# Splitting q and k after the transpose instead of before it, and storing the last output tiles one by one

## The chip, the core and the metric

The kernel runs on one core of one Trainium2 chip. The metric is the device time of one execution in microseconds (us). A core has five engines that run their own instruction streams and meet on semaphores: TensorE (PE, matrix products and transposes), VectorE (DVE), ScalarE (ACT), GpSimd (POOL) and SyncE (SP, which here only issues transfers). SBUF is the on-chip memory with 128 partitions, PSUM the eight banks into which PE writes.

## What is computed

A block-causal attention, then a mixture of eight experts with a skip test, then a two-layer MLP, all in float32:

```python
def _attn_ref(q, k, v):            # 4 batches, 8 heads, 576 tokens, 64 dims a head
    scores = scale * np.matmul(q, k.transpose(0, 1, 3, 2))
    scores = np.where(block_i >= block_j, scores, -1000000000.0)   # blocks of 64
    scores = scores - np.max(scores, axis=-1, keepdims=True)
    attn = np.exp(scores)
    attn = attn / (np.sum(attn, axis=-1, keepdims=True) + 1e-09)
    return np.matmul(attn, v)
...
# x = attention output, 2304 tokens x 512
# experts: out = x, or x + gate * relu(x @ w1[e]) @ w2[e] where x @ w_skip > 0
# MLP: g = max(h, 0) + alpha * min(h, 0), h = x @ w_in (512 x 2048);  out = g @ w_out
```

## The kernel before, in words

The 32 heads are taken as 16 pairs of heads. A pair has nine units (`UNITS`): four query tiles of 128 tokens of each of the two heads (`FULL`), and a joint unit (`JOINT`) for the last 64 queries of both heads (`TAIL`). A unit is scores on PE (L739 and the mask at L741, or L733 for the joint one), a maximum on DVE (L1117), an exponential on ACT (L976), transposes of the probabilities on PE (L751) and a copy of them on DVE (L1131, L1128). Once a pair, PE multiplies with v (L762, L768) for the pair before and turns the output back to rows (L786); DVE sums up (L1137 to L1142) and scales.

Scores need near-float32 precision from a PE format that rounds (`F32R`). So q and k are split into a rounded part (high) and the rest (low), and each score is two products of depth 128: high and low parts of one head are stacked on the two halves of the partitions, keys as (high, low), queries once as (high, low) and once swapped as (low, high).

Before the change, GpSimd splits q and k **as loaded**, tokens on partitions (`split_pair`: additions of zero at L579 give the high part, subtractions at L583 the low part), into `parts`, where each tile of each head is 64 columns high and 64 columns low. PE transposes these 128x128 tiles (`qk_chunk`, L715 for full tiles, L711 for the tails), 18 in a pair: 4 of q and 4 of k for each head, and 2 tails. They come in the five chunks of `CHUNKS`, at units 2, 3, 3, 5 and 6 of the pair ahead of the one that uses them (`QK_AT`), into a ring of three PSUM banks (`RING`, in the order of `ORDER`) shared with the transposed probabilities. ACT copies them out (`qk_out`, L962 to L967) into `q_t` and `k_t`. The swapped queries are made by SP with transfers from SBUF to SBUF (`swap`, L417), four in a pair of 160 KB each.

The order on every engine is written out by hand: `pair(n, par)` on PE, ACT and DVE. SP's queue has in each step (`load_step(n)`) the loads of q and k for pair n+2 (six transfers), the swaps of head 0 of pair n+1, the three loads of v, the swaps of head 1, and behind them one transfer each that zeroes, saves finished rows (in the later steps) and loads expert weights (in the first eight steps). SP waits in that order, so what stands behind a waiting transfer waits too.

The MLP goes in six chunks of three tiles. At its end, `project` signals `g_used` after the last nine products (L931), ACT copies three tiles (`out_rows`, L1095) and SP stores them (L536, L540).

## Time and profile before

| what | us |
|---|---|
| median of 3 runs (lowest, highest) | 872.41 (871.15, 872.70) |
| the profiled execution | 871.87 |
| its span, first to last instruction | 870.0 |
| attention stage (scores of all 16 pairs), about | 0 to 234 |
| routing, about | 234 to 255 |
| experts, about | 255 to 430 |
| MLP, about | 430 to 870 |
| PE busy in the span | 817.1 |
| DVE, ACT, POOL busy | 446.4, 274.5, 190.4 |

The busy times of the engines overlap. A pair of the attention stage takes 13.7 us, so the stage is sixteen nearly equal periods with a start and an end.

### The profile page before, as it was taken

How to read it: one execution, taken by the hardware profiler on the slowest of the kernel's cores; microseconds unless marked ns; L12 is line 12 of the kernel's file. 1: busy time of each engine (PE TensorE's matmuls, PEld its weight loads, DVE VectorE, ACT ScalarE, POOL GpSimd, SP SyncE). 2: the span in 40 equal slices, each digit the busy share in tenths (PEclk: the TensorE clock that was granted, in tenths of full speed). 3: DMA queues.
4: the chain of work that ended last, by engine and by line, in shares of the span. 5: the costliest groups of instructions: out<-in, count | busy, mean ns of one | idle time of the engine just before them, and what ended most of it. 6: DMA issues, size and time to landing. Idle time of an engine off the chain costs nothing.

```text
span 870.0 us, 15697 instructions
## 1 busy us (share of the span) xinstructions
PE 817.1 (94%) x5281; PEld 721.9 (83%) x5282; DVE 446.4 (51%) x916; ACT 274.5 (32%) x650; POOL 190.4 (22%) x191
## 2 busy tenths in 40 slices
PE   5999999999749999999769999999999999999997
PEld 4788888888549989989659889989998998998996
DVE  3777777777874444226544734543544434444432
ACT  5666665666333333133311121111112112112111
POOL 6242424422011143014178810000001001000000
PEclk9999999999959999999969999999999999999999
DMA  6678888675417766149433110002002002000001
GB/s 140 160 188 222 215 229 234 164 208 166 141 39 242 273 234 227 50 169 323 148 108 99 60 44 29 0 2 70 0 0 72 0 0 72 0 0 36 1 1 37
DMA packets 94599, 95.76 MB, mean 110 GB/s; under 512 B 64112, under 2 KB 65264, under 8 KB 94064
## 3 DMA queue, kind: packets, MB, share of 16 engines
q1 hardware_dynamic: 86000, 67.65, 27.4%
q0 software_dynamic: 4208, 14.95, 5.8%
q10 hardware_dynamic: 4368, 12.88, 4.0%
q8 instruction: 12, 0.20, 0.1%
q14 instruction: 11, 0.09, 0.0%
HBM read 64.78 MB, written 20.19 MB: 98 GB/s over the span
## 4 chain that ended last, share of the span: by engine, by line
PE 86%; DVE 4%; DMA 3%; ACT 3%; issue 2%; POOL 0%; SPq 0%; ACTq 0%; DVEq 0%; POOLq 0%
PE bank L920 23%; PE bank L931 22%; PE bank L870 9%; PE bank L884 8%; PE bank L751 6%; PE bank L762 4%; PE bank L739 3%; PE bank L715 2%; PE bank L733 2%; PE bank L786 2%; DMA w_sb<-in_moe_w_dram 1%; ACT p_sb L976 1%; PE bank L768 1%; PE bank L908 1%; PE bank L857 1%
## 5 line engine op out<-in xcount | busy, mean ns | idle before, releaser
L1412 DVE TENSOR_SCALAR g_sb<-bank,alpha_sb 128x384 f32<-128x384 f32 x96 | 59.3, 618 | 218.7 <-PE bank L920 218.6
L1088 ACT CAST g_hi<-g_sb 128x384 fp32r<-128x384 f32 x96 | 49.5, 515 | 321.8 <-DVE g_sb L1414 321.8
L920 PE MATMUL bank<-u_hi,wi_hi 128*128 128x384 f32 x384 | 130.5, 340 | 1.4 <-DVE u_lo L1385 1.4
L920 PE MATMUL bank<-u_hi,wi_lo 128*128 128x384 f32 x384 | 130.4, 340 | 0.0
L920 PE MATMUL bank<-u_lo,wi_hi 128*128 128x384 f32 x384 | 130.0, 339 | 0.0
L931 PE MATMUL bank<-wo_lo,g_hi 128*128 128x512 f32 x288 | 113.7, 395 | 0.0
L931 PE MATMUL bank<-wo_hi,g_lo 128*128 128x512 f32 x288 | 113.5, 394 | 0.0
L931 PE MATMUL bank<-wo_hi,g_hi 128*128 128x512 f32 x288 | 112.7, 391 | 0.8 <-DVE g_lo L1418 0.8
L870 PEld LDWEIGHTS bank<-rows_t,w_sb 128*128 128x128 f32 x832 | 97.6, 197 | 2.6 <-DVE rows_t L1329 1.5
L870 PE MATMUL bank<-rows_t,w_sb 128*128 128x128 f32 x832 | 97.9, 280 | 1.1 <-DVE rows_t L1329 1.1
L976 ACT ACTIVATE p_sb<-bank,neg_max 128x128 f32<-128x128 f32 (+2 forms) x144 | 79.1, 551 | 48.6 <-DVE neg_max L1117 46.1
L1117 DVE TENSOR_REDUCE neg_max<-bank 128x1 f32<-128x128 f32 (+2 forms) x144 | 72.5, 511 | 33.4 <-PE bank L733 19.3
L920 PEld LDWEIGHTS bank<-u_hi,wi_hi 128*128 128x128 f32 x384 | 73.0, 190 | 5.4 <-DVE u_lo L1385 1.8
L920 PEld LDWEIGHTS bank<-u_lo,wi_hi 128*128 128x128 f32 x384 | 72.9, 190 | 3.6
L920 PEld LDWEIGHTS bank<-u_hi,wi_lo 128*128 128x128 f32 x384 | 72.9, 190 | 0.0
L751 PE MATMUL bank<-ident,p_sb 128*128 128x128 f32 x400 | 69.3, 285 | 1.8 <-DVE p_t L1131 0.3
L739 PE MATMUL bank<-k_t,q_t 128*128 128x128 f32 (+3 forms) x256 | 68.0, 358 | 2.2 <-DMA q_t<-q_t 1.4
L1131 DVE COPY p_t<-bank 128x128 f32<-128x128 f32 (+3 forms) x128 | 60.6, 484 | 14.6 <-PE bank L751 12.9
L660 POOL DMA_INDIRECT u_sb<-y_slots,from_i x18 | 18.2, 1010 | 227.8 <-PE bank L908 214.4
L931 PEld LDWEIGHTS bank<-wo_lo,g_hi 128*128 128x128 f32 x288 | 54.0, 188 | 11.6
L931 PEld LDWEIGHTS bank<-wo_hi,g_hi 128*128 128x128 f32 x288 | 54.1, 188 | 10.4 <-issue 1.3
L931 PEld LDWEIGHTS bank<-wo_hi,g_lo 128*128 128x128 f32 x288 | 54.0, 188 | 9.1
(171 smaller groups left out, 1230.2 us busy)
## 6 DMA issues: line engine op xcount, KB each, us to landing
w_sb<-in_moe_w_dram ACTq DMA_DIRECT2D x6, 2048.0 KB, 8.0
w_sb<-in_moe_w_dram SPq DMA_DIRECT2D x6, 2048.0 KB, 10.8
q_t<-q_t SPq DMA_DIRECT2D x64, 160.0 KB, 2.5
w_sb<-in_moe_w_dram SPq DMA_DIRECT2D x16, 512.0 KB, 4.8
v_nat<-in_v_dram SPq DMA_DIRECT2D x32, 128.0 KB, 2.4
y_out<-in_moe_w_out_dram POOLq DMA_DIRECT2D x16, 256.0 KB, 3.0
out_dram<-y_out SPq DMA_DIRECT2D x16, 256.0 KB, 2.8
qk_nat<-in_q_dram SPq DMA_DIRECT2D x30, 128.0 KB, 4.0
```

The lines of the kernel that those rows point to most:

```text
L739: pe.matmul(a[:, 0:keys], q_t[:, par, z, h, P * (i + 1):P * (i + 2)], k_t[:, par, h, 0:keys], start=z == 0, stop=False)
L751: last = pe.transpose(t[:, P * j:P * j + P], p_sb[:, c % PB, P * j:P * j + P], ident[:])
L762: last = pe.matmul(O_MAIN[HALF * h:HALF * h + HALF, P * unit:MAIN], v_nat[:, unit, h, :], p_t[:, h, unit, P * unit:MAIN], start=unit == 0, ...
L870: last = pe.matmul(HIDDEN[c][:, P * z:P * z + P], w1_sb[:, par, j, P * f:P * f + P], rows_t[:, j, :], start=j == 0, stop=j == KD - 1)
L884: last = pe.matmul(RESULT, h[:, f, :], w, start=f == 0 and z == 0, stop=f == KF - 1 and z == 2)
L920: last = pe.matmul(dst, w[:, j, P * f:P * f + P], u[:, j, :], start=z == 0, stop=z == len(terms) - 1)
L931: last = pe.matmul(YBANK[i][:, :], g[:, f % GB, P * i:P * i + P], w[:, f, :], start=f == 0 and z == 0, stop=f == FI - 1 and z == 2)
L976: act.activation(p_sb[:, c % PB, 0:keys], scores_ap(c), ACT.Exp, bias=neg_max[:, c:c + 1], accum_out=row_sum[:, par, i, h:h + 1]).then_inc ...
L1088: act.copy(g_hi[:, f % GB, :], g_sb[:, f % 2, :]).then_inc(g_hi_done, 1)
L1117: dve.reduce_max(neg_max[:, c:c + 1], scores_ap(c), AX.X, negate=True).then_inc(max_done, 1)
L1131: dve.tensor_copy(p_t[:, h, 0:i + 1, P * i:P * i + P], t[:, 0:P * (i + 1)].rearrange("p (j c) -> p j c", c=P)).then_inc(pt_evac, 1)
L1412: dve.tensor_scalar(g, a, 0.0, alpha_sb[:, f:f + 1], ALU.min, ALU.mult).then_inc(neg_done, 1)
```

## The change

q and k are transposed as they are loaded: a 128x128 tile holds both heads, 64 columns each, so a pair has 9 transposes (4 of q, 4 of k, 1 for the tails), in three chunks at units 2, 3 and 5. They are made two pairs ahead. ACT copies them as plain float32 into `raw_t`; GpSimd then splits them there, a pair ahead, one head at a time on the 64 partitions of that head (four instructions of 64x1152), into `qk_t`. SP brings the missing halves over: for each head first the high part of q (64x576), then the low parts of q and k (64x1152). Pair 0 is split by ACT and DVE directly from PSUM. `qk_nat` gets two buffers, `parts` goes. In the last MLP chunk PE signals after each tile's three products, ACT copies each tile when it is ready, and ACT itself issues the last half tile's store.

```diff
-        CHUNKS = [(0, 0), "tails", (0, 1), (1, 0), (1, 1)]
+        CHUNKS = ["q", "k", "tails"]
...
-        QK_AT = [2, 3, 3, 5, 6]
+        QK_AT = [2, 3, 5]
+        GAP_AT = [3, 6]
...
+            def swap(n, par, h):
+
+                sp.wait_ge(hi_done, 2 * n - 1 + h)
+                sp.dma_start(columns(other(h), n, LOW_AT[h], S).bitcast(F32), high(n, h)[:, 0:S].bitcast(F32)
+                             ).then_inc(swapped[par][h], 16)
+                sp.wait_ge(lo_done, 2 * n - 1 + h)
+                sp.dma_start(columns(other(h), n, HIGH_AT[h], 2 * S).bitcast(F32), low(n, h).bitcast(F32)
+                             ).then_inc(swapped[par][h], 16)
+
+            def load_step(n, par, more=True):
+
+
+                if more:
+                    sp.wait_ge(qk_tr, QC * n + QC)
+                    load_qk(n + 3, 1 - par)
+                swap(n + 1, 1 - par, 0)
                 sp.wait_ge(pv_done, 2 * n)
                 load_v(n)
-                swap(n + 1, (1,))
+                swap(n + 1, 1 - par, 1)
...
             first_load(sp, 0, q_h)
-            load_qk(1, first_nat, second_loaded)
+            load_qk(1, 1)
+            swap_first(0)
+            load_half(2, 0, 0)
+            swap_first(1)
+            load_half(2, 1, 0)
             sp.wait_ge(v_zero, 1)
             load_v(0)
-            swap(0)
-            sp.wait_ge(first_split, 2)
-            load_qk(2, qk_nat, qk_loaded)
-            swap(1)
+            sp.wait_ge(qk_tr, QC)
+            load_qk(3, 1)
+            swap(1, 1, 0)
+            swap(1, 1, 1)
...
+            def split_pair(n, par, second=False):
+
+                pool.wait_ge(qk_evac, QC * n)
+                if not second:
+                    pool.wait_ge(s_done, UNITS * (n - 1))
+                for h in range(2):
+                    src = raw_t[own(h), par]
+                    pool.tensor_tensor(high(par, h), src, zero_c[own(h), :].to_broadcast([HALF, 2 * S]), ALU.add).then_inc(hi_done, 1)
+                    pool.wait_ge(hi_done, 2 * n - 1 + h)
+                    pool.tensor_tensor(low(par, h), src, high(par, h).bitcast(F32), ALU.subtract).then_inc(lo_done, 1)
...
+            def turn(src, c, t):
+
+                tiles = {"q": range(FULL), "k": range(FULL, 2 * FULL), "tails": [2 * FULL]}[CHUNKS[c]]
+                for i, z in enumerate(tiles):
+                    last = pe.transpose(t[:, P * i:P * i + P], src[:, z].rearrange("p h d -> p (h d)"), ident[:])
+                return last
...
+            def project_end(c):
+
+                f = FI - 1
+                pe.wait_ge(g_lo_done, FI * c + FI)
+                for i in range(CH):
+                    for z, (g, w) in enumerate(((g_hi, wo_hi), (g_lo, wo_hi), (g_hi, wo_lo))):
+                        last = pe.matmul(YBANK[i][:, :], g[:, f % GB, P * i:P * i + P], w[:, f, :], start=False, stop=z == 2)
+                    last.then_inc(last_done, 1)
```

**PE in the middle of a pair (units 2 and 3).** In the rows, bank and bank_4 are banks of the ring, `parts` is what GpSimd split, `p_sb` the probabilities, `k_t,q_t` the operands of the scores. Before:

```order
L715 MATMUL bank<-ident,parts 128x128 x4
L739 MATMUL bank_2<-k_t,q_t 128x256 x2
L741 MATMUL bank_2<-mask_r,mask_l 128x64
L749 REGISTER_ALU
L751 MATMUL bank_4<-ident,p_sb 128x128 x4
L711 MATMUL bank_4<-ident,parts 128x128 x2
L702 ISA
L715 MATMUL bank<-ident,parts 128x128 x4
```

The same place in the changed kernel, where L759 is the transpose of the loaded q and k and L793, L795, L805 are the former L739, L741, L751:

```order
L759 MATMUL bank<-ident,qk_nat 128x128 x4
L793 MATMUL bank_2<-qk_t 128x256 x2
L795 MATMUL bank_2<-mask_r,mask_l 128x64
L803 REGISTER_ALU
L805 MATMUL bank_4<-ident,p_sb 128x128 x4
L759 MATMUL bank_4<-ident,qk_nat 128x128 x4
```

The two tail transposes have left this place, one has gone to unit 5, and the chunks of four at units 5 and 6 are gone.

**GpSimd, one pair.** Before:

```order
L579 TENSOR_TENSOR parts<-qk_nat,zero_c 128x8x64
L579 TENSOR_TENSOR parts<-qk_nat,zero_c 128x10x64
L581 REGISTER_ALU
L583 TENSOR_TENSOR parts<-qk_nat,parts 128x8x64
L583 TENSOR_TENSOR parts<-qk_nat,parts 128x10x64
```

In the changed kernel the four instructions of a pair have 1152 columns each on 64 partitions:

```order
L628 TENSOR_TENSOR qk_t<-raw_t,zero_c 64x1152
L629 ISA
L630 TENSOR_TENSOR qk_t<-raw_t,qk_t 64x1152
L628 TENSOR_TENSOR qk_t<-raw_t,zero_c 64x1152
L630 TENSOR_TENSOR qk_t<-raw_t,qk_t 64x1152
```

The columns that go through the engine rise from 2304 to 4608 a pair.

**SP at the start of the program**, from the load of v for pair 0 to the swaps of pair 1. Before (the first L417 row is pair 0's four swaps, the second pair 1's):

```order
L401 DMA v_nat<-in_v_dram 128x4x64 x2
L404 DMA v_nat<-in_v_dram 64x2x64
L417 DMA q_t<-q_t 64x640 x4
L393 DMA qk_nat<-in_q_dram 128x4x64 x2
L396 DMA qk_nat<-in_q_dram 64x2x64
L393 DMA qk_nat<-in_k_dram 128x4x64 x2
L396 DMA qk_nat<-in_k_dram 64x2x64
L417 DMA q_t<-q_t 64x640 x4
```

In the changed kernel, from pair 0's swaps of head 1 (L445, L448) to pair 1's of head 0 (L454, L457); ahead of it stand the swaps of head 0 and pair 2's load of q:

```order
L445 DMA qk_t<-qk_t 64x576
L448 DMA qk_t<-qk_t 64x576
L424 DMA qk_nat<-in_k_dram 128x4x64 x2
L427 DMA qk_nat<-in_k_dram 64x2x64
L436 DMA v_nat<-in_v_dram 128x4x64 x2
L439 DMA v_nat<-in_v_dram 64x2x64
L424 DMA qk_nat<-in_q_dram 128x4x64 x2
L427 DMA qk_nat<-in_q_dram 64x2x64
L424 DMA qk_nat<-in_k_dram 128x4x64 x2
L427 DMA qk_nat<-in_k_dram 64x2x64
L454 DMA qk_t<-qk_t 64x576
L457 DMA qk_t<-qk_t 64x1152
```

Pair 1's swaps now stand behind the loads of two more pairs and of v.

## Rows read from the trace of the kernel before

**Rows 1.** Busy time by stretch: start:end, length, busy us of each engine (instructions), clock, DMA share, GB/s.

```profile
94.80:108.50 13.70, 13.61 (x124) 11.35 (x122) 9.96 (x28) 8.76 (x27) 5.05 (x4) 1.00 0.88 227
```

**Rows 2.** The chain that ended last, one pair: start us, us, what.

```profile
121.74 2.35 PE bank L762 x16
...
125.73 0.44 PE bank L715 x4
...
126.92 0.23 PE bank L711 x2
...
129.16 0.44 PE bank L715 x4
129.59 1.29 PE bank L733 x8
...
131.24 0.44 PE bank L715 x4
...
135.46 2.35 PE bank L762 x16
```

**Rows 3.** GpSimd by form, 45 to 205 us: count, busy us, mean ns, idle before.

```profile
L583 POOL TENSOR_TENSOR parts<-qk_nat,parts 128x640 fp32r<-128x640 f32 x12 | 18.6, 1549 | 0.0
...
L579 POOL TENSOR_TENSOR parts<-qk_nat,zero_c 128x640 fp32r<-128x640 f32 x12 | 15.0, 1253 | 0.0
```

**Rows 4.** Timeline of GpSimd at the start: start us, us, engine, line, operation.

```profile
1.74 0.14 POOL L554 MEMSET mask_l<- 1x64 bf16 x1
...
1.82 0.14 POOL L555 MEMSET mask_r<- 128x64 bf16 x1
```

**Rows 5.** The chain that ended last, at the start of the program.

```profile
5.59 0.86 DVE parts L1209
...
7.31 1.10 PE bank L715 x4
...
10.07 2.59 DMA q_t<-q_t
...
12.80 0.41 PE bank L739 x2
```

**Rows 6.** Timeline of SP and PE at the start (SPq is SP's queue issuing transfers).

```profile
12.38 1.19 SPq L393 DMA_DIRECT2D qk_nat<-in_q_dram  x2
...
15.11 0.42 PE L739 MATMUL bank<-k_t,q_t 128*128 128x128 f32 x2
...
22.02 0.42 PE L739 MATMUL bank<-k_t,q_t 128*128 128x128 f32 x2
```

**Rows 7.** Timeline of SP over one period.

```profile
100.46 1.28 SPq L417 DMA_DIRECT2D q_t<-q_t  x2
...
111.70 1.36 SPq L396 DMA_DIRECT2D qk_nat<-in_k_dram  x1
```

**Rows 8.** Busy time of one microsecond in which swaps of rows 7 run.

```profile
102.00:103.00 1.00, 1.00 (x9) 0.88 (x7) 0.28 (x1) 0.79 (x2) 0.71 (x1) 1.00 0.95 220
```

**Rows 9.** Timeline of the end.

```profile
864.35 1.56 ACT L1095 COPY y_out<-bank 128x512 f32<-128x512 f32 x3 [4.41 <-PE bank L931]
864.96 0.33 SPq L536 DMA_DIRECT2D out_dram<-y_out  x1
865.45 2.40 SPq L540 DMA_DIRECT2D out_dram<-y_out  x4
```

**Rows 10.** Single DVE lines: count, duration ns min/median/max, first and last start us.

```profile
L1398 DVE SCALAR_TENSOR_TENSOR u_sb<-u_sb,gate,x_tok x15: 740/747/2017, 482.6 to 762.3; 128x512 f32<-128x512 f32 x15
```

**Rows 11.** Timeline of GpSimd and DVE in one pair.

```profile
131.95 2.77 POOL L583 TENSOR_TENSOR parts<-qk_nat,parts 128x512 fp32r<-128x512 f32 x2
...
137.33 0.15 DVE L1137 TENSOR_SCALAR sum_eps<-row_sum 128x8 f32<-128x8 f32 x1
...
138.77 0.62 DVE L1131 COPY p_t<-bank 128x128 f32<-128x128 f32 x2 [0.81 <-PE bank L751]
```

**Rows 12.** Busy time in one microsecond of routing.

```profile
237.00:238.00 1.00, 0.00 (x0) 0.00 (x0) 0.90 (x4) 0.00 (x0) 0.00 (x0) 0.65 0.00 0
```

**Rows 13.** The chain that ended last, two experts' first layers.

```profile
255.22 10.24 PE bank L870 x64
...
271.50 7.14 PE bank L870 x64
```

More of the change, by code:

```diff
@@ L43, in program @@
     NAT = 2 * FULL + 1
-    QW = P + MAIN
     UNITS = 2 * FULL + 1
@@ L375, in program, with turns, own, other @@
         SAVED = 16 * ((B - 1) * FULL + B - 1 + 4)
+        FIRST_BANKS = [bank[7], bank[3], bank[2]]
+        SECOND_BANKS = [bank[5], bank[6], bank[4]]
+        def turns(n):
+            return not isinstance(n, int) or n + 2 < PAIRS
+        def own(h):
+            return slice(HALF * h, HALF * h + HALF)
+        def other(h):
+            return slice(HALF - HALF * h, P - HALF * h)
+        def columns(rows, n, at, count):
+            if isinstance(n, int):
+                return qk_t[rows, n % 2, at:at + count]
+            return qk_t[rows, bass.ds(n % 2, 1), at:at + count].rearrange("p a s -> p (a s)")
+        def high(n, h):
+            return columns(own(h), n, HIGH_AT[h], 2 * S)
+        def low(n, h):
+            return columns(own(h), n, LOW_AT[h], 2 * S)
         def first_load(queue, z, src):
             for h in range(2):
-                queue.dma_start(qk_nat[:, FULL * z:FULL * z + FULL, h, :],
+                queue.dma_start(first_nat[:, FULL * z:FULL * z + FULL, h, :],
                                 src[h:h + 1, 0:MAIN, :].rearrange("a (t p) d -> p (a t) d", p=P)
                                 ).then_inc(first_loaded[z], 16)
-            queue.dma_start(qk_nat[TAIL * z:TAIL * z + TAIL, 2 * FULL, :, :],
+            queue.dma_start(first_nat[TAIL * z:TAIL * z + TAIL, 2 * FULL, :, :],
                             src[0:2, MAIN:S, :].rearrange("h p d -> p h d")).then_inc(first_loaded[z], 16)
@@ L537, in _ @@
                     else:
-                        for z in range(2):
+                        for z in range(1 if t == T_TILES - 1 else 2):
                             b = 2 * (t - B * FULL) + z
@@ L558, in _ @@
             pool.memset(o_t[:, S:], 0.0).then_inc(ident_0, 1)
-            for h in range(2):
-                pool.memset(q_t[:, :, 0, h, HALF - HALF * h:P - HALF * h].bitcast(F32), 0.0).then_inc(ident_0, 1)
+            for at in (HIGH_AT[1], LOW_AT[1]):
+                pool.memset(qk_t[:, :, at - HALF:at].bitcast(F32), 0.0).then_inc(ident_0, 1)
             pool.memset(w_route[:], 0.0).then_inc(route_zero, 1)
@@ L815, in _ @@
             pair(0, 0, first=True)
-            with pe.Fori(1, PAIRS - 1, 2) as n:
+            with pe.Fori(1, PAIRS - 3, 2) as n:
                 pair(n, 1)
                 pair(n + 1, 0)
+            pair(PAIRS - 3, 1)
+            pair(PAIRS - 2, 0)
             pair(PAIRS - 1, 1, last=True)
@@ L994, in pair @@
                     for j, at in enumerate(QK_AT):
-                        if at == c - 1 and not last:
+                        if at == c - 1 and turns(n):
                             qk_next(j, n, par)
@@ L1000, in _ @@
             act.activation(warm[:], zero_c[:], ACT.Exp)
-            act.wait_ge(first_loaded[0], 48)
-            act.wait_ge(first_loaded[1], 48)
-            act.copy(parts[:, 0, FULL:, :, 0:DH], qk_nat[:, FULL:]).then_inc(first_hi, 1)
+            first_high()
+            for c in range(QC):
+                qk_out(c, 1, 1, SECOND_BANKS[c])
             act.wait_ge(const_ready, 1)
-            for c in range(QC):
-                qk_out(c, 0, 0, RING[(c - QC) % 3])
             pair(0, 0, first=True)
-            with act.Fori(1, PAIRS - 1, 2) as n:
+            with act.Fori(1, PAIRS - 3, 2) as n:
                 pair(n, 1)
                 pair(n + 1, 0)
+            pair(PAIRS - 3, 1)
+            pair(PAIRS - 2, 0)
             pair(PAIRS - 1, 1, last=True)
@@ L1095, in out_rows, with last_rows @@
                     act.copy(y_out[:, i, :], YBANK[i][:, :]).then_inc(out_evac, 1)
+            def last_rows(c):
+                act.wait_ge(wo_split, FI)
+                act.wait_ge(out_stored, 16 * CH * c + 16)
+                for i in range(CH):
+                    act.wait_ge(last_done, i + 1)
+                    act.copy(y_out[:, i, :], YBANK[i][:, :]).then_inc(out_evac, 1)
+                act.wait_ge(out_evac, CH * c + 2 * CH)
+                act.dma_start(out[B * S - TAIL:B * S, :], y_out[P - TAIL:P, CH - 1, :]).then_inc(last_stored, 16)
             def mlp_step(c, last):
@@ L1206, in _ @@
             dve.sem_inc(head_part_done, 1)
[L1208 to L1215 removed]
+            for h in range(2):
+                dve.wait_ge(first_hi, 2 * h + 1)
+                for lo, hi, src in ((TAIL, S, FIRST_BANKS[0][:, 0:MAIN]), (0, TAIL, FIRST_BANKS[2][:, 0:TAIL])):
+                    last = dve.scalar_tensor_tensor(low(0, h)[:, lo:hi], src[own(h)], SCALE, high(0, h)[:, lo:hi].bitcast(F32),
+                                                    ALU.mult, ALU.subtract)
+                last.then_inc(first_lo, 1)
+                dve.wait_ge(first_hi, 2 * h + 2)
+                k_low = columns(other(h), 0, HIGH_AT[h] + S, S)
+                for lo, hi, src in ((TAIL, S, FIRST_BANKS[1][:, 0:MAIN]), (0, TAIL, FIRST_BANKS[2][:, TAIL:2 * TAIL])):
+                    last = dve.tensor_tensor(k_low[:, lo:hi], src[own(h)], high(0, h)[:, S + lo:S + hi].bitcast(F32), ALU.subtract)
+                last.then_inc(first_lo, 1)
             dve.wait_ge(ones_ready, 1)
```

266 lines of the change are left out of this document (130 added, 136 removed).

## The prediction

> **What bounds the kernel now.** I read the busy time by stretch first. In a period of the attention stage PE is busy for 13.61 of 13.70 us, DVE for 9.96, ACT for 8.76, GpSimd for 5.05, and the transfer engines for 0.88 of the time at 227 GB/s [rows 1]. So PE sets the pace, and the nearest second is not an engine but the transfers: 0.88 of 13.7 is 12.1 us. Then the chain that ended last: from one product with v to the next it takes 135.46 - 121.74 = 13.72 us, and nearly all pieces in between are PE's [rows 2]. The work that the change removes lies on that chain: four pieces of four transposes at 0.44 us and one of two at 0.23, in all 18 transposes for 1.99 us, 0.11 each [rows 2]. (Busy sums give 0.15 each; that counts overlapping instructions twice, the chain does not.) Last, SP's timeline: the first swap of a period is issued at 100.46, the last load before the next one ends at 111.70 + 1.36 = 113.06 [rows 7], so SP's own work in a period is 12.6 us of 13.7. Behind PE at 13.7 stand transfers at 12.1 and SP at 12.6; that is what the change has to fit into.
>
> **The change, part by part.** I follow the moment at which PE starts the scores of a pair, from pair 0 to pair 15, and add the end.
>
> *Start, up to the scores of pair 0.* Before: q has landed at 5.59, then come DVE's two splits, transposes, ACT, SP and a transfer that lands 2.59 us after 10.07, and scores start at 12.80 [rows 5]. Now the transposes come first. Four take 1.10 us there (against 0.44 later) [rows 2, 5], so q and tails are turned at about 6.9. ACT copies 512 columns in about 0.52 (three in 1.56) [rows 9] and twice 64 columns in, I take, 0.2 each (no row; between 0 and 0.52): 7.8. DVE subtracts 512 columns in 0.74 at two SBUF or PSUM inputs [rows 10] and 64 in 0.2: 8.75. SP issues the low part then, and it lands 2.6 us later [rows 5]: scores of pair 0 at about 11.5, 1.3 us earlier.
>
> *From pair 0 to pair 1.* PE reached head 1 of pair 0 at 15.11 and pair 1 at 22.02 [rows 6]. Without waits that would be 13.8 and, with nine transposes less (0.99), 19.7. But SP is late. A load costs it 0.6 us (two in 1.19) [rows 6], a swap 0.64 (two in 1.28) [rows 7]. From 9.5, when pair 0's head 0 has been issued, the new order has three loads of q (1.9 with gaps), two swaps (1.3), three loads of k (1.9), v (1.8), six loads of pair 3 (3.8), which ends at 20.2. Head 1's swap of pair 0 lands at about 14.6 instead of 13.8 (0.8 late). Pair 1's swap of the low parts is issued at 20.9 and lands 2.6 us later, and 0.65 more since it is 295 KB instead of 160 (at 220 GB/s [rows 8], 0.61): 24.1. GpSimd is not what is late: pair 1 has been copied out at about 11.4, and head 0 is split 5.1 us later. So PE, ready at 20.5, waits 3.6 us, and pair 1's scores start at 24.2 instead of 22.02: **2.2 us later**.
>
> *From pair 1 to pair 15.* Before, 14 intervals had 18 transposes each, 252. Now 13 pairs make 9 each, 117, since the last interval has none. 135 times 0.11 [rows 2] is **14.9 us**. ACT also loses two copies of 512 columns in a pair, and DVE nothing, so neither comes closer. The new interval is 13.7 - 0.99 = 12.7 us.
>
> *GpSimd.* Its four instructions of 512 and 640 columns become four of 1152. Per column they cost 1253/640 = 1.96 ns (addition) and 1549/640 = 2.42 ns (subtraction) [rows 3], so 2.26 and 2.79 us, 10.1 in a pair and about 10.4 with three waits between. That they have 64 partitions instead of 128 helps nothing: a fill of 64 columns takes 0.14 us on 1 partition and on 128 [rows 4]. Bounds: 5.05 if partitions counted after all, 13.9 if each took 3.4 us; I take 10.4, by the nearest rows. It starts when the joint scores of two pairs before are done and is needed one interval later, so 10.4 in 12.7 leaves 2.3 us, less what SP does behind it.
>
> *SP and the transfers.* The number of transfers in a step is the same. Swapped bytes rise from 4 x 160 KB to 2 x (147 + 295) = 885 KB (655 before): at 220 GB/s [rows 8] 4.0 instead of 3.0 us. So the transfers need 12.1 + 1.0 = 13.1 us of a 12.7 us interval in the eight steps with weights. Against that: head 0's swap is issued some 6.7 us after an interval begins (1.3 late start from the cycle, 4.7 of loads, 0.7) and lands at about 10, 2.7 us before it is needed. Eight times 0.4 makes 3.2 us of lag against 2.7 of slack. Bounds: 0 if the transfers overlap better, 8 x 1.0 - 2.7 = 5.3 if those eight intervals stay at 13.7. I take **1.0 us**. After the eighth step nothing of weights is left.
>
> *Routing, experts, MLP* are untouched and start earlier with it.
>
> *The end.* ACT's first copy starts at 864.35 and takes 0.52; SP issues one store at 864.96 and four from 865.45 to 867.85 [rows 9], and the span ends 2.15 us after that, at 870.0. Now the three tiles are ready 1.4, 0.7 and 0 us before 864.35. SP issues the first store at about 863.6, the next two behind it, and the first half of the last tile at 865.5 to 866.1; ACT issues the other half at 865.0. The end is at 866.1 + 2.15 = 868.25: **1.75 us earlier**.
>
> *Sum*: +2.2 - 14.9 + 1.0 - 1.75 = -13.4 us. Against the profiled execution, 871.87, that is 858.5; against the median, which is 0.5 higher, 859.0. I forecast 859.0.
>
> **Rivals.**
>
> *A. The queues keep the eight weight steps near the old pace.* For it: 13.1 us of transfers for 12.7, and SP at 12.6. Against it: landing has slack, and SP's cycle had a wait in it. It gives the upper bound above, 4.3 us more than taken: 863.5.
>
> *B. The small DVE sums wait for GpSimd.* In one pair GpSimd is done at 134.72 and L1137 runs at 137.33 [rows 11]; so the two never ran together before. Now GpSimd is at work for 10.4 us from the end of the joint scores (129.59 + 1.29 = 130.88 [rows 2]), and L1137 comes 6.0 us after that point, inside the third instruction, which ends at 7.5. That DVE can be held up beside GpSimd is in the trace: L1398 takes 740 ns and once 2017 [rows 10]. If L1137 waits 1.5 us, 0.8 of it is covered by the idle time ahead of L1131 [rows 11], and up to 0.7 goes on PE's path, some 0.4 after what later work absorbs; 14 times 0.4 is 5.6: 864.5. The Trainium skill, SBUF — State Buffer, section "Who interferes with whom", says that a DVE tensor_scalar between SBUF operands can take a port pair that it shares with GpSimd and that the second to come then waits the whole instruction out. By that rule the time would be 864.5, and no row of before shows this instruction beside GpSimd.
>
> *C. GpSimd sets the pace, slower than before.* If an instruction on half the partitions, out of a plain contiguous row, costs over 3.35 us instead of 2.5, GpSimd's pair passes 13.7 us and the gain is gone; at 4.0 us the pair takes 16.4, and 14 times 2.7 us more than 13.7, less the end, gives about 910. Likewise if all the small sums wait for the fourth instruction. Against it: the per-column prices of four forms agree [rows 3].
>
> *D. PE's clock falls while PE waits for pair 1.* In routing the granted clock is 0.65 over a microsecond in which PE does nothing [rows 12]: in it, the clock goes from 2.4 GHz to 1.2. The wait forecast above is 3.6 us. The price is that of coming back: the first 64 products after routing take 10.24 us, the same ones later 7.14 [rows 13], so 3.1 us: 862.
>
> *E. Pair 1 does not wait*, since SP's start is quicker than I add up: 3.6 us less, 855.5.
>
> **How the numbers follow.** Chances: the forecast 0.45 (its own range 856.5 to 861.5), A 0.15, B 0.13, C 0.05, D 0.10, E 0.12. The range of 80% runs from 853.5 (E, and no lag) to 866 (A or B, with some of the other); what is left out is C and combinations. About 0.2% (1.7 us) is what a measurement of this kernel can tell from no change. All cases but C are faster by more than that; for errors that I do not see, I put faster at 0.92, same at 0.03, slower at 0.05.
>
> **What would show it.** In the changed profile: nine transposes a pair at 0.11 on the chain, and 12.7 us from one product with v to the next; GpSimd's forms of 64x1152 at 2.26 and 2.79 us; pair 0's scores at 11.5 and pair 1's at 24.2, with PE idle ahead of them for a transfer of `qk_t`; transfers busy over 0.95 in the weight steps and PE's intervals in them up to 13; L1137 at 0.15 us (against B); the last store issued at about 4 us before the end. The prediction is wrong if intervals stay above 13.2 throughout, if GpSimd's instructions are over 3.3 us, or if PE waits for more than the one swap.

## The result, and the profile after

The changed kernel takes 865.8 us (median of 4 runs, 864.2 to 866.7) against 872.6 for the kernel before (4 runs): ratio 0.9923, 95% interval 0.9903 to 0.9943, so 6.8 us less, where 13.4 were forecast (859.0, with a range of 853.5 to 866, at whose upper edge the result lies). Its profiled execution took 866.7 us with a span of 864.9.

First the stretches of one ordinary period, of the period that came out long, of the eight steps with weights, and of the microseconds in which the clock was down (columns as in [rows 1]):

```profile
88.25:101.40 13.15, 12.88 (x112) 10.20 (x112) 10.73 (x29) 7.58 (x26) 9.49 (x4) 1.00 0.91 230
114.67:130.53 15.86, 13.37 (x113) 10.23 (x113) 12.12 (x29) 7.68 (x26) 9.47 (x4) 1.00 1.05 231
30.63:140.15 109.52, 105.17 (x910) 82.73 (x907) 88.14 (x219) 61.85 (x196) 74.73 (x33) 1.00 1.00 235
25.00:26.00 1.00, 1.00 (x7) 0.69 (x5) 1.00 (x3) 0.42 (x2) 1.00 (x1) 0.51 0.21 9
27.00:28.00 1.00, 1.00 (x4) 0.35 (x5) 0.74 (x2) 0.41 (x2) 1.00 (x1) 0.50 0.79 180
```

An ordinary period is 13.15 us, 0.55 under that of [rows 1] and 0.45 over the forecast of 12.7. PE is no longer busy throughout (12.88 of 13.15). GpSimd works 9.5 us, and the transfers are busy for 1.00 of the time in the weight steps. The same stretch of the kernel before:

```profile
32.00:141.00 109.00, 108.27 (x964) 90.40 (x964) 79.50 (x216) 69.55 (x207) 39.57 (x32) 1.00 0.84 217
```

I follow the start of the joint scores (L786, before L733) from pair to pair. Before, pair 0 is at 19.93 us, pair 1 at 33.35, pair 15 at 224.53. After: 18.55, 35.34, 221.19. So the start gave 1.4 us, pair 1 took back 3.4, and the fourteen intervals behind it gave 5.3 where 12.9 to 13.9 had been forecast (14.9 less 1.0 counted from scores to scores; 12.9 counted from joint scores to joint scores, since the last such interval had no transposes before either). After, they are ten of 13.15 to 13.27, one of 15.86 (pair 8), one of 13.08, and the last two, in which nothing is turned any more, 12.39 and 12.36.

**Start.** Rows of the timeline of PE and then of SP in the changed kernel, against [rows 5, 6]:

```profile
10.47 0.41 PE L793 MATMUL bank<-qk_t 128*128 128x128 f32 x2 [1.42 <-DMA qk_t<-qk_t]
18.55 1.44 PE L786 MATMUL bank<-qk_t 128*128 128x512 f32 x8
23.45 0.44 PE L793 MATMUL bank<-qk_t 128*128 128x128 f32 x2 [3.10 <-DMA qk_t<-qk_t]
...
15.62 1.14 SPq L424 DMA_DIRECT2D qk_nat<-in_q_dram  x2
18.65 0.61 SPq L427 DMA_DIRECT2D qk_nat<-in_k_dram  x1
19.95 0.59 SPq L457 DMA_DIRECT2D qk_t<-qk_t  x1
```

Pair 1's low parts (288 KB here, the 295 KB of the prediction: 294,912 bytes) are issued at 19.95, behind the six loads of pair 3, and PE waits 3.10 us for them. Behind that wait the granted clock is 0.50, the lower of its two levels (1.2 GHz), for some 3.5 us.

**The chain within a pair.** First, rows of the chain that ended last in the kernel before that belong between 126.92 and 129.16 of [rows 2]:

```profile
127.17 0.04 ACT q_t L962
127.35 0.26 ACT k_t L963
128.09 0.58 ACT p_sb L976 x2
128.72 0.44 PE bank L751 x2
```

From 127.15 to 128.72 the chain went through ACT, and one of the four pieces of L715 is not on it: [rows 2] has three (125.73, 129.16, 131.24). With the two of L711 that is 14 transposes for 1.55 us on the chain, where the prediction counted 18 for 1.99. The same detour stands in other pairs (at 44.91, 72.33, 99.76 and 168.31).

Timeline of the kernel before, PE and then ACT, from the turned q to the joint scores:

```profile
166.70 0.60 PE L715 MATMUL bank<-ident,parts 128*128 128x128 f32 x4
168.11 0.60 PE L715 MATMUL bank<-ident,parts 128*128 128x128 f32 x4
168.47 0.59 PE L739 MATMUL bank<-k_t,q_t 128*128 128x384 f32 x2
170.48 0.82 PE L733 MATMUL bank<-k_t,q_t 128*128 128x512 f32 x3
...
167.34 0.60 ACT L965 ACTIVATE q_t<-bank 128x512 fp32r<-128x512 f32 x1 [0.40 <-PE bank L715]
167.83 0.36 ACT L976 ACTIVATE p_sb<-bank,neg_max 128x128 f32<-128x128 f32 x1
169.73 0.58 ACT L976 ACTIVATE p_sb<-bank,neg_max 128x384 f32<-128x384 f32 x1
```

The same in the changed kernel (PE, its weight loads, ACT, DVE):

```profile
166.42 0.65 PE L759 MATMUL bank<-ident,qk_nat 128*128 128x128 f32 x4
167.66 0.60 PE L759 MATMUL bank<-ident,qk_nat 128*128 128x128 f32 x4
168.20 0.61 PE L793 MATMUL bank<-qk_t 128*128 128x384 f32 x2
170.21 1.07 PE L786 MATMUL bank<-qk_t 128*128 128x512 f32 x5 [0.26 <-ACT p_sb L1056]
...
168.20 0.30 PEld L793 LDWEIGHTS bank<-qk_t 128*128 128x128 f32 x2 [0.17 <-ACT p_sb L1056]
...
167.20 0.60 ACT L1045 ACTIVATE raw_t<-bank 128x512 f32<-128x512 f32 x1 [0.58 <-PE bank L759]
167.69 0.36 ACT L1056 ACTIVATE p_sb<-bank,neg_max 128x128 f32<-128x128 f32 x1
169.49 0.58 ACT L1056 ACTIVATE p_sb<-bank,neg_max 128x384 f32<-128x384 f32 x1
...
168.90 0.56 DVE L1208 TENSOR_REDUCE neg_max<-bank 128x1 f32<-128x384 f32 x1 [0.34 <-PE bank L795]
```

What to see: from the start of q's transposes to the joint scores it is 170.48 - 166.70 = 3.78 us before and 170.21 - 166.42 = 3.79 after, although PE has five transposes fewer in between. ACT copies the turned q (0.6) ahead of the exponential of unit 4; scores 6 go into the bank that this exponential frees; then come maximum 6 on DVE, exponential 6 on ACT, and the joint scores, whose banks that one frees. Before, PE had just enough to do to hide this chain; now it waits 0.17 and 0.26 us in it. The transposes taken from unit 6, outside the chain, did pay: the interval fell by 13.71 - 13.25 = 0.46 us, and from the start of the joint scores to the next scores (L739, L793) it is 158.85 - 156.77 = 2.08 us before and 158.53 - 156.96 = 1.57 after.

**The long period.** SP, PE, DVE and GpSimd in the changed kernel:

```profile
111.87 0.59 SPq L457 DMA_DIRECT2D qk_t<-qk_t  x1
...
117.72 0.43 PE L793 MATMUL bank<-qk_t 128*128 128x128 f32 x2 [1.23 <-DMA qk_t<-qk_t]
126.73 0.65 PE L759 MATMUL bank<-ident,qk_nat 128*128 128x128 f32 x4 [0.99 <-DVE p_t L1222]
...
123.62 2.31 DVE L1228 TENSOR_SCALAR sum_eps<-row_sum 128x8 f32<-128x8 f32 x1
...
121.10 2.10 POOL L628 TENSOR_TENSOR qk_t<-raw_t,zero_c 64x1152 fp32r<-64x1152 f32 x1
123.28 2.63 POOL L630 TENSOR_TENSOR qk_t<-raw_t,qk_t 64x1152 fp32r<-64x1152 f32 x1
```

The swap of head 0 takes 5.7 us to land and PE waits 1.23 us for it. That delay moves DVE's addition of eight numbers a row into GpSimd's fourth instruction. It ends at 125.93, when GpSimd does (125.91), and PE waits another 0.99 us for the copy behind it.

**The end**, against [rows 9]. ACT and SP:

```profile
859.08 1.87 ACT L1182 COPY y_out<-bank 128x512 f32<-128x512 f32 x3 [3.12 <-PE bank L998]
859.69 0.33 SPq L588 DMA_DIRECT2D out_dram<-y_out  x1
860.29 1.79 SPq L592 DMA_DIRECT2D out_dram<-y_out  x3
860.97 0.57 ACTq L1184 DMA_DIRECT2D out_dram<-y_out  x1
```

The last product starts at 859.93, so 4.97 us lie between it and the end; before it was 870.0 - 863.93 = 6.07.

### The profile page after: what moved, and what is told of

Read it like the earlier page. It is cut to its first block, busy times and chain, and to the rows that moved or that the text cites. A ratio compares the mean times of both kernels' runs of the same rounds, so it can differ in the third digit from the quotient of the medians.

```text
span 864.9 us, 15180 instructions
## 1 busy us (share of the span) xinstructions
PE 808.3 (93%) x5137; PEld 704.2 (81%) x5138; DVE 459.7 (53%) x921; ACT 256.8 (30%) x621; POOL 258.1 (30%) x191
## 4 chain that ended last, share of the span: by engine, by line
PE 80%; SPq 6%; DVE 5%; issue 3%; DMA 3%; POOL 2%; ACT 1%; DVEq 0%; POOLq 0%
PE bank L977 23%; PE bank L988 22%; PE bank L927 11%; PE bank L941 8%; PE bank L805 3%; PE bank L816 3%; PE bank L793 2%; PE bank L840 2%; PE bank L786 2%; SPq L427 1%; SPq L424 1%; PE bank L759 1%; DVE neg_max L1208 1%; DMA qk_t<-qk_t 1%; POOL qk_t L628 1%
## 5 line engine op out<-in xcount | busy, mean ns | idle before, releaser
L630 POOL TENSOR_TENSOR qk_t<-raw_t,qk_t 64x1152 fp32r<-64x1152 f32 x30 | 79.2, 2640 | 2.4
L628 POOL TENSOR_TENSOR qk_t<-raw_t,zero_c 64x1152 fp32r<-64x1152 f32 x30 | 63.0, 2101 | 55.8 <-PE bank L786 50.2
L793 PE MATMUL bank<-qk_t 128*128 128x128 f32 (+3 forms) x256 | 70.2, 367 | 5.7 <-DMA qk_t<-qk_t 5.7
L805 PE MATMUL bank<-ident,p_sb 128*128 128x128 f32 x400 | 70.0, 287 | 0.7 <-DVE p_t L1222 0.6
L988 PEld LDWEIGHTS bank<-wo_lo,g_hi 128*128 128x128 f32 x285 | 53.4, 187 | 11.5
```

What stands on the lines that cost most here:

```text
L628: pool.tensor_tensor(high(par, h), src, zero_c[own(h), :].to_broadcast([HALF, 2 * S]), ALU.add).then_inc(hi_done, 1)
L630: pool.tensor_tensor(low(par, h), src, high(par, h).bitcast(F32), ALU.subtract).then_inc(lo_done, 1)
L793: pe.matmul(a[:, 0:n_keys], qk_t[:, par, at + TAIL + P * i:at + TAIL + P * i + P], qk_t[:, par, keys:keys + n_keys], start=at == HIGH_AT[h ...
L805: last = pe.transpose(t[:, P * j:P * j + P], p_sb[:, c % PB, P * j:P * j + P], ident[:])
L988: last = pe.matmul(YBANK[i][:, :], g[:, f % GB, P * i:P * i + P], w[:, f, :], start=f == 0 and z == 0, stop=f == FI - 1 and z == 2)
```

## The experiments

Each kernel was timed in turn with the kernel before. "Joint scores of pair 9" is the moment at which the attention stage leaves the weight steps (143.80 in the changed kernel).

**1. ACT's copies later.**

```diff
+        COPY_AT = [4, 5, 6]
...
-                        if at == c - 1 and turns(n):
+                        if at == c and turns(n):
```

> The changed kernel, with only ACT's order altered: the copy of the turned q comes behind the exponential of unit 4 instead of ahead of it, the copy of k behind that of unit 5. My theory is a chain through ACT: turned q, its copy (0.6 us), exponential 4, scores 6 (same bank), maximum 6, exponential 6, joint scores, 3.8 us in both kernels. By it scores 6 no longer wait (0.17 us now) and an interval falls from 13.25 to about 13.1 us, 1.5 to 2 us in all. Rival, PE's own work or SP's queue sets the interval: it stays at 13.2 and the time within 0.5 us of the changed kernel's.

864.5 us, ratio 0.9906 (0.9889 to 0.9922). Ordinary intervals are 12.96 to 13.05 instead of 13.15 to 13.27, as the chain has it. The total is about 1.5 us under the changed kernel's, as expected, but the two ratios' intervals overlap; three intervals of 13.6 and one of 15.68 stand among the others, with waits for late swaps.

**2. The transposes of k between scores 6 and the joint scores.**

```diff
-        QK_AT = [2, 3, 5]
+        QK_AT = [2, 4, 5]
+        COPY_AT = [4, 6, 6]
```

> The changed kernel with the transposes of k at unit 4 instead of 3, so behind scores 6 and ahead of the joint scores, and ACT's copies at 4, 6, 6. By the theory of the chain through ACT, scores 6 start 0.5 us earlier against the rest, the 0.26 us wait of the joint scores is filled with work that is there anyway, and an interval is 12.85 us: 13 times 0.4, about 5 us less (861). Rival, SP and the transfers hold the weight steps: only the five intervals behind them gain, 2 us. Rival, nothing was waiting and the transposes only cost what they cost: no change.

864.0 us, ratio 0.9899 (0.9884 to 0.9915), where 861 was expected. The intervals are as the chain has them: 12.81 to 12.93, in weight steps too. PE and ACT rows of its timeline:

```profile
125.73 0.60 PE L760 MATMUL bank<-ident,qk_nat 128*128 128x128 f32 x4
126.84 0.59 PE L794 MATMUL bank<-qk_t 128*128 128x384 f32 x2
127.87 0.66 PE L760 MATMUL bank<-ident,qk_nat 128*128 128x128 f32 x4 [0.25 <-DVE p_t L1223]
129.15 0.76 PE L787 MATMUL bank<-qk_t 128*128 128x512 f32 x3
...
126.11 0.37 ACT L1057 ACTIVATE p_sb<-bank,neg_max 128x128 f32<-128x128 f32 x1
126.46 0.59 ACT L1046 ACTIVATE raw_t<-bank 128x512 f32<-128x512 f32 x1
```

The exponential of unit 4 now comes ahead of the copy, and 3.79 us have become 129.15 - 125.73 = 3.42. But there are two intervals of 15.5 where the changed kernel has one of 15.86, and the clock is down for 6 us behind a wait of 3.79 at pair 1. So the 13.2 is explained; the long intervals are another matter.

**3. Pair 1's first swap ahead of pair 3's loads.**

```diff
-            sp.wait_ge(qk_tr, QC)
-            load_qk(3, 1)
             swap(1, 1, 0)
+            sp.wait_ge(qk_tr, QC)
+            load_qk(3, 1)
             swap(1, 1, 1)
```

> The changed kernel with pair 1's first two swaps issued ahead of the six loads for pair 3. If SP's order at the start is the reason for PE's 3.1 us wait, pair 1's scores start at about 20.4 us instead of 23.45. If the wait is what drops the granted clock to 0.50 for 3.5 us behind it, that stretch disappears too, worth 1.7 us more: 4.8 us in all. If the clock drop has another cause: 3.1 us only. If loads of pair 3 come late instead: a new wait at unit 2 of pair 1.

Pair 1's scores start at 20.12 without a wait, the clock stays at 1.00, pair 1's joint scores are at 31.35 instead of 35.34: 4.0 us gained there. From scores to joint scores pair 1 takes 11.23 with a wait of 0.66 for ACT in it, so 10.57, against 11.89 behind the wait: the clock's part was 1.3 us. And then most of it is lost again: pair 2's interval is 15.85 and pair 9's 15.96, and pair 9 is at 143.15. At pair 2 PE waits 1.35 us ahead of its scores; the profile puts it down to ACT, but the exponential that frees their bank had ended at 32.2, and it is the swap, issued at 30.97 and landing 3.4 us later, that fits the 34.51 at which PE went on. In the changed kernel SP issued it at 30.63, hardly earlier; it was not late there because PE came 4.0 us later. The time is 866.1, ratio 0.9925 (0.9907 to 0.9943), that of the changed kernel. The expectation did not have this.

**4. The addition of 1e-9 with a tensor operand.**

```diff
-                dve.tensor_scalar(sum_eps[:, 0:FULL, :], row_sum[:, par, 0:FULL, :], 1e-9, None, ALU.add)
+                dve.tensor_tensor(sum_eps[:, 0:FULL, :], row_sum[:, par, 0:FULL, :], eps_c[:], ALU.add)
```

> The changed kernel with the 128x8 addition of 1e-9 on DVE as a tensor plus tensor (a constant tile) instead of tensor plus number. Theory: the number form waits for GpSimd's instruction that is running (about 1.0 us a pair, once 2.3), the tensor form does not or does as well; DVE has room for it in ordinary pairs, so the interval stays 13.2 and the time falls by at most 1 us (the pair where it reached PE). Rival, DVE's wait is a part of the 13.2: the interval falls by 0.3 and the time by 4 us.

It waits just the same: 143, 1088 and 2380 ns (least, median, most), against 150, 1097 and 2314 for the form with a number. 867.5 us, ratio 0.9947 (0.9925 to 0.9968): no gain.

**5. Half of w2's loads spread over the next four steps.**

```diff
-                sp.dma_start(w2_sb[:, e, ...], w2_v[e][...])      # in each of eight steps
+                if i is not None:                                 # in every second one
+                    load_w2(e, i)
...
                 rest_step(2 * n2 + 1, 1, True)
+                load_w2(0, n2 - 2)
                 rest_step(2 * n2 + 2, 0, True)
+                load_w2(1, n2 - 2)
```

> The changed kernel with half of the w2 loads (four of 512 KB) taken out of the eight weight steps and put one each into the four steps behind them. Theory: in the eight weight steps the transfers (busy 1.00 of the time at 235 GB/s) set a period of 13.7 us against PE's 13.2, the lag ends in one late swap of 1.2 us and a DVE wait of 1.0 behind it. By it the joint scores of pair 9 come 106 to 106.5 us after those of pair 1 instead of 108.5, no swap is late, and the time falls by 2 to 2.5 us. Rival, SP's own instructions are the limit (13 transfers at 0.6 us with waits in line): half an instruction less a step, 0.3 us, so 108. Rival, the late swap is an accident of one place: it stays.

864.7 us, ratio 0.9909 (0.9894 to 0.9924). From pair 1 to pair 9 it took 108.46 us, the same as in the changed kernel; the one late interval (15.97) only came five pairs earlier, at pair 3, in the second step. Its swap was issued at 43.98 (43.84 in the changed kernel), and PE was 1.4 us earlier there. That told against my account of a slow lag over eight steps.

**6. All weights issued by ACT.** ACT issues the two loads behind exponential 0; SP has two transfers less a step.

> The changed kernel with all sixteen expert-weight loads issued by ACT behind exponential 0 (where ACT idles 2.4 us), at the same rate; SP has two transfers less a step, the bytes are the same. If SP's line of instructions sets 13.7 us in the weight steps, its period falls to 13.2, pair 9's joint scores come 106 us behind pair 1's and the time falls by 2.5 us. If the transfers set it (my theory), 108 to 109 stays and the time is within 1 us of the changed kernel's, or worse, since the weights now land ahead of the swaps.

869.8 us (864.9 to 873.4 in twelve runs), ratio 0.9961 (0.9941 to 0.998), by the medians 4 us slower than the changed kernel, though the two intervals just touch. In the profile, which is of the slowest of the twelve, four swaps behind pair 1's are late, up to 2.81 us; the 288 KB swap lands in 7.6 us (median) against 4.3. Two issues less a step on SP gained nothing. The Trainium skill, DMA: Bandwidth & Descriptors, section "Issuing engines are not separate DMA queues", says that transfers started by different engines share the same 16 DMA engines and interleave, so that only issuing time is saved; this case agrees (the engines were busy for 1.08 of the time, and the swaps landed later).

**7 and 8. The kernel before with transposes left out.** Seven leaves out five at units 3 and 5 of each pair, eight leaves out three of four at unit 6; the output, and with it the routing, is another, so only intervals are read, from one run each.

```diff
-                    for i in range(FULL):
+                    for i in range({2: FULL - 1, 3: FULL - 3}.get(c, FULL)):     # and one tail of two (7)
+                    for i in range(FULL if c < 4 else 1):                        # (8)
```

> The kernel before, leaving out in each pair five transposes of the middle chunks (one of two tails and one of four of q at unit 3, three of four of k at unit 5), the places at which the change makes fewer; the output differs and with it the routing, so only the interval from joint scores to joint scores is read. If each transpose on PE counts as I summed, the interval falls from 13.71 by five times 0.09 to 0.11, to 13.2. By the theory of the chain through ACT (3.8 us from the turned q to the joint scores), it falls by 0.2 at most, to 13.5 or above.

> The kernel before, leaving out three of the four transposes at unit 6 in each pair, outside that chain; again only the interval is read. Both theories: three times 0.09, 13.44 us. If it stays at 13.7, something else than PE and the chain sets the interval.

Five transposes fewer in the middle took the interval from 13.71 to 13.61, 0.02 each. Its joint scores (timeline of PE):

```profile
157.71 1.56 PE L733 MATMUL bank<-k_t,q_t 128*128 128x512 f32 x8
171.33 0.84 PE L733 MATMUL bank<-k_t,q_t 128*128 128x512 f32 x3
```

Three fewer at unit 6 made 13.55, 0.05 each, where both theories had 13.44. The row of the one that is left there:

```profile
158.00 0.27 PE L715 MATMUL bank<-ident,parts 128*128 128x128 f32 x1
```

From its start to that of the next scores (158.17) it takes 0.17 us, where the four take 158.85 - 158.50 = 0.35. From joint scores to scores it is 1.91 us, between the 2.08 of before and the 1.57 of the changed kernel, which has none there. So the price was wrong outside the chain too: it is not proportional to the number, and going by the changed kernel the last one is worth the most. The chain was there before the change, and PE's count of transposes did not price it.

**9. The end alone, on the kernel before.** The edit is that of `project_end`, `last_rows` and the store by ACT.

> The kernel before with only the end of the change: in the last chunk a signal after each tile's three products, each tile copied when ready, ACT issuing the last half tile's store. Forecast: 1.75 us less. From the two traces: 6.07 us from the start of the last product to the end became 4.97, so 1.1 us less, 871.7 against 872.8.

871.4 us, ratio 0.9983 (0.9975 to 0.9992): 1.5 us less, 0.7 to 2.2. In its own trace 869.5 - 864.79 = 4.7 us lie between the last product and the end, 1.4 less than before.

**10. No weights in the attention stage**, with pair 1's swap first; they are loaded behind it.

> The changed kernel with pair 1's swap first (as before) and with all sixteen expert-weight loads moved behind the attention stage; the experts start late and only the attention stage is read. If the transfers of the weight steps are what holds pairs 1 to 9, the swaps never come late: pair 1's joint scores at 31.35 us, then 13.2 us each, pair 15's at 214.5 instead of 221.2, transfers busy under 0.85 of the time. If the swaps are late by themselves (GpSimd, SP's order), one interval of 15.9 stays and pair 15 is at 217 or later.

Behind pair 2 no swap is late, all intervals are 13.2, and the transfers are busy for 0.74 of the time. Pair 2 is late all the same (15.87, with PE waiting 1.39 us ahead of its scores as in experiment 3, and 0.81 for DVE); pair 15 is at 217.6. That is what the second expectation said (one interval of 15.9, pair 15 at 217 or later), while everything behind pair 2 is what the first said. (It is one run; the experts then start late: 871.3 us.) So something else than the weights makes pair 2's swap late, and the weights have a part in the later ones: experiment 3, with the same order and the weights, had 15.96 at pair 9 too. Pair 2's low parts are issued at 30.99 here, at 30.97 in experiment 3.

**11. The sums at unit 5.**

```diff
-        PV_AT, O_AT, SUMS_AT, ROWS_AT = 0, 2, 0, JOINT
+        PV_AT, O_AT, SUMS_AT, ROWS_AT = 0, 2, 5, JOINT
```

> The changed kernel with DVE's small sums at unit 5 of a pair instead of unit 0, where GpSimd has finished. If they wait only for a GpSimd instruction that is running, the 128x8 addition takes 0.15 us in every pair again. DVE had room at unit 0, so an ordinary interval stays 13.2; the 1.0 us that PE waits for DVE behind a late swap disappears, and the time falls by 1 to 1.5 us. Rival, the addition waits at unit 5 too: no change, or slower, since it is then on the way to the joint scores.

The addition takes 157 to 171 ns in every pair, and PE's 0.99 us wait is gone; two late swaps cost 0.6 and 1.4 us instead of one of 2.6. Pair 15 is at 219.95 (221.19). 865.6 us, ratio 0.9918 (0.9903 to 0.9933): the difference of 1 us is seen in the trace, not told by the times.

**12 to 17. Combinations, to find what makes a swap late.** Twelve has edits 2, 3, 5 and 11.

> The changed kernel with four edits together: k turned at unit 4 with ACT's copies at 4, 6, 6 (fills the wait of the joint scores), pair 1's swap first, the sums at unit 5, and half of w2's loads spread over the next four steps. By the sum of my causes: pair 1's joint scores at 31.0, then 12.85 us each to pair 13 if the transfers allow it (pair 15 at 210, the time near 855); if the transfers of the first steps still hold it, they set pair 9 at about 141 and the time is 860.

860.3 us, ratio 0.9866 (0.9848 to 0.9884). Intervals of 12.8, but 15.81 and 14.06 at pairs 2 and 3 and two of 13.4 and 13.6 later; pair 9 at 137.7.

Thirteen has edit 3 and head 0's swap ahead of the six loads in every step; fourteen adds edits 2 and 11, fifteen also edit 5.

```diff
+                swap(n + 1, 1 - par, 0)
                 if more:
                     sp.wait_ge(qk_tr, QC * n + QC)
                     load_qk(n + 3, 1 - par)
-                swap(n + 1, 1 - par, 0)
```

> The changed kernel with one alteration of SP's order in every step: head 0's swap of the next pair ahead of the six loads for three pairs on, not behind them (pair 1's too). The bytes are the same. If the late swaps come from their place behind loads that are needed much later, every swap of head 0 is issued 3 to 4 us earlier, none is late, all intervals are 13.2 (pair 1 at 31.35, pair 9 at 137, pair 15 at 214.5) and the time is 859 to 860. If the transfers' throughput sets the weight steps, the lag moves to the loads: a wait of PE's transposes for qk_nat or of v, and pair 9 stays at 141 to 143.

> The one before this, with k turned at unit 4 (ACT's copies at 4, 6, 6) and DVE's sums at unit 5; the weights as in the changed kernel. If place in the order was the cause, 12.8 us each: pair 9 at 30.4 + 8 x 12.8 = 133, pair 15 at 209, the time near 853. If throughput is near: in the weight steps the transfers need 13.2 to 13.7 us and some wait comes back, pair 9 at 137 to 140, the time 857.

> The one before this, with half of w2's loads spread over the four next steps. Only if throughput limits the version without it does this one gain: then pair 9 at 133 to 135 and 1 to 3 us less than it; otherwise the same time.

All three are slower than the kernel before: 881.1 (1.0095, 1.0071 to 1.0119), 877.6 (1.0068, 1.0047 to 1.009) and 878.4 (1.0068, 1.0052 to 1.0084). Rows of thirteen, SP and PE:

```profile
97.12 0.51 SPq L528 DMA_DIRECT2D w_sb<-in_moe_w_dram  x1
97.96 0.40 SPq L529 DMA_DIRECT2D w_sb<-in_moe_w_dram  x1
98.50 0.49 SPq L454 DMA_DIRECT2D qk_t<-qk_t  x1
99.03 0.59 SPq L457 DMA_DIRECT2D qk_t<-qk_t  x1
105.57 3.04 SPq L427 DMA_DIRECT2D qk_nat<-in_k_dram  x1
...
109.07 0.43 PE L793 MATMUL bank<-qk_t 128*128 128x128 f32 x2 [3.06 <-DMA qk_t<-qk_t]
```

The swap is now right behind 1 MB of weights and has the loads beside it: it lands 9.9 us after it is issued. The six loads ahead of the swap were a spacer, as I read it, and not an obstacle. Only pair 2 gained (intervals 12.78 and 13.19 there).

Sixteen is twelve with the four small loads of the routing weights issued by ACT, so that SP's first step begins 3 us earlier; seventeen is twelve without edit 5.

> The kernel with the four edits of the earlier combination (swaps behind the loads again), and the four small loads of the routing weights issued by ACT (two after the copies of pair 1, two after pair 0), where SP issued them ahead of its first step (22.5 to 26.1). SP's first step then starts 3 us earlier. The wait of 2.7 us for pair 2's swap should fall to 0.5 or nothing; if the transfers of the first steps do not allow more, it comes back as a longer wait at pair 3. ACT's issues may cost up to 1 us at pair 0. Expected: pair 9's joint scores at 135 to 137 instead of 137.7, the time 1 to 2.5 us under that of the earlier combination (858 to 859); the same, if a later swap takes the wait over.

> The same combination as the earlier one without the spreading of w2's loads (and with SP's small loads where they were): k at unit 4, pair 1's swap first, sums at unit 5. With all weights in the eight steps the transfers need 13.2 to 13.7 us a step against PE's 12.8. If throughput matters there: pair 9's joint scores at 140 to 143 instead of 137.7, and the time 2 to 4 us above the earlier combination's 860.3. If bytes do not matter: the same.

Sixteen takes 859.0 us, ratio 0.9863 (0.9844 to 0.9882), the lowest of all, though the times do not tell it from twelve. From pair 0 to pair 11 every interval is 12.68 to 12.85, pair 9 is at 135.2. The stretch from pair 1's joint scores to pair 10's, with PE busy for 113.03 of 115.27 us:

```profile
32.70:147.97 115.27, 113.03 (x1011) 91.07 (x1010) 88.47 (x244) 70.04 (x217) 85.49 (x36) 1.00 1.01 232
```

Pair 2's low parts are issued at 28.27 instead of 30.95, and pair 2 no longer waits: that was the start's part, SP's own line of instructions. The transfers are busy for 1.01 of the time here and no swap is late behind pair 0, so that share alone does not make one late. Seventeen takes 865.5, ratio 0.9913 (0.9899 to 0.9928): in its profile (869.4 us, the slowest of six) there are swap waits of 7.8 us in four places behind pair 0's, up to 2.97 each, and pair 9 is at 148.3, where 140 to 143 was expected. At 12.8 us a pair, taking four loads out of the weight steps is worth 5 us by the medians, 4 by the ratios; at 13.2 it was worth nothing that shows (experiment 5).

## Why the prediction was wrong, step by step

**The failed step is "135 times 0.11 is 14.9 us", with "the new interval is 13.7 - 0.99 = 12.7 us".** It priced each transpose by its time on the chain of [rows 2], wherever it stood, and it misread that chain: 14 transposes are on it, not 18, and for 1.6 us it runs through ACT. The reading that "nearly all pieces in between are PE's" passed over the very place. PE's row of pieces ran side by side with a second chain through ACT and DVE that was equally long between unit 2 and the joint scores (3.78 us). Of the nine transposes taken from a pair, five lay inside it and gave next to nothing: shown by the two timelines, and by experiment 7 (five for 0.10 us). The four at unit 6 gave 0.46, as 0.11 each would make it, but not in equal parts: three of them gave 0.16 (experiment 8). Reordering ACT (experiments 1, 2) brought the interval to 13.0 and 12.85, which is nearly the forecast's 12.7. That "ACT loses two copies and comes no closer" was true of its busy time and beside the point: its place in the chain counted, not its sum. Ten intervals at 0.5 us over 12.7 are 5 us of the missing gain.

**SP and the transfers, "I take 1.0 us", was too small.** By its own sum (3.2 of lag less 2.7 of slack) the prediction had 0.5. Transfers went from 0.84 of 13.71, 11.5 us a pair (the prediction's 12.1 was one period's 0.88), to 1.00 of 13.7: 2.2 us more, where 1.0 was forecast. The bytes were right (217 x 13.71 = 2.98 MB, now 235 x 13.69 = 3.22), the price of them was not: I had put it at the rate of 220 GB/s. Why they cost more is not shown. Rival A was right in kind. The form is a late swap in one place, 15.86 - 13.2 = 2.7 us with what follows, inside the bounds of 0 to 5.3. That the weight transfers have a part in the later ones follows from experiments 10 (without weights none behind pair 2) and 17 against 12, and 6 fits (same bytes by another engine: not better). At pair 2 it is SP's line of instructions at the start (30.97, 30.99 and 30.95 in experiments 3, 10 and 12, and 28.27 in 16, where the wait is gone). In my first account a slow lag over eight steps led to the late swap; experiment 5 contradicts that, since it came in the second step. What fits all runs is that PE may run ahead of SP's steps only so far, and whatever it gains at the start or by shorter intervals is given back at a later swap, unless SP's steps come earlier (16) or carry fewer weights (12 against 17). Why it is this swap and not the next is open.

**Rival B happened as written, its price did not.** The addition waits for GpSimd in most pairs (median 1.10 us), and DVE has room for it. It reached PE only behind the late swap, for 0.99 us. The Trainium skill, SBUF — State Buffer, section "Who interferes with whom", says that a DVE instruction with both inputs in SBUF also contends with GpSimd's reads; experiment 4 agrees (2380 ns at most), and 11 shows the way out, another moment.

**Rival D happened, smaller.** PE waited 3.10 us and the clock fell; it cost 1.3 us (experiment 3), not 3.1. Rival E did not: pair 1 waited. Of the signs that the prediction named against itself, one came in full, PE waiting for more than the one swap (1.23 us at 117.72); the ordinary intervals, 13.15 to 13.27, lie on either side of the 13.2 of another.

**Right:** the start (scores of pair 0 at 10.47 for 11.5 and of pair 1 at 23.45 for 24.2, the wait 3.10 for 3.6, and its cause, which experiment 3 shows), GpSimd's two forms (2.10 and 2.64 us for 2.26 and 2.79; half the partitions save nothing) and with it the end of rival C, and that routing, experts and MLP stay as they were (from pair 15's joint scores to the end 643.7 us for 645.5, of which the end is 1.1). The end was put at 1.75 us; the two traces give 1.1, experiment 9 gives 1.5 and its interval holds both.

The sum over the attention stage: forecast for pair 15, 224.53 + 2.2 - 13.9 = 212.8; measured 221.2; experiment 16, in which both failed terms are mended, 212.2. That these two agree so closely is partly luck: the forecast had a wait of 3.6 us at pair 1 in it that experiment 16 does not have, and sixteen has pair 0's joint scores 1.5 us later.

## What to carry to other kernels

Where an engine is busy for 99% of a period, a second chain can be just as long beside it: before pricing a removed instruction, follow the latencies from each buffer's release to the next use through the other engines, and count only what lies outside. The instruction order on an engine that is 60% busy may be what sets the pace.

Transfers that are hidden at one pace can be the bound at the next: what is gained ahead of a queue that is full can be given back at its next urgent transfer. Take bytes out of the crowded steps first; moving the urgent transfer forward can put it behind something worse. And read the whole chain that ended last, the short pieces of other engines too: here they stood in it before the change.

## What the runs showed that I had not expected

A swap's landing time depends on its neighbours far more than on its size: the 288 KB swap took 3.6 us (median) without weights, 4.3 in the changed kernel (where the one of half its size took 3.7), 7.6 with weights issued by ACT, and 9.9 once right behind two weight loads.

The granted clock also fell early, at about 11 us, in the changed kernel and in eight of fourteen experiments of its form (0.52 to 0.73 on average over 11 to 16 us), and in none of four profiles in the form of before. Changed kernel:

```profile
6.00:11.00 5.00, 3.33 (x20) 2.72 (x18) 3.30 (x8) 3.98 (x12) 0.64 (x2) 1.00 0.67 152
11.00:16.00 5.00, 5.00 (x29) 3.81 (x29) 3.53 (x9) 2.84 (x9) 4.84 (x3) 0.66 0.76 174
```

Where it lasted until 18 to 21 us, pair 0's joint scores came at 20.0 to 21.3 instead of 17.9 to 18.9 (19.9 in one without a fall). What decides it is open. Nor does a wait's length alone: in experiment 13 PE waits 3.06 us up to 109.07 and the clock stays at 1.00 behind it, and 3.07 us up to 125.57, where it is 0.50. The kernel before varies there too, without the clock: 19.9 to 22.2 us in four profiles. The one that I forecast from was the earliest of them, which is part of why the traces differ by 5.1 us and the medians by 6.8.
